# Moving two matmul groups of an expert's second layer behind a vote of the routing search

## The reference

```python
def _moe_ref(x, w_gate, w1, w2):
    ...
    logits = x @ w_gate
    order = np.argsort(-logits.flatten())
    for idx in order:
        tok, e = (int(idx) // E, int(idx) % E)
        if assigned[tok] >= 0 or counts[e] >= cap:
            continue
        assigned[tok] = e
        counts[e] += 1
    ...
    for e in range(E):
        mask = assigned == e
        h = np.maximum(x[mask] @ w1[e], 0.0)
        out[mask] = h @ w2[e]
```

## Time and profile before

| | |
|---|---|
| median of 3 runs | 1320.37 us (1319.72 to 1323.32) |
| profiled execution: its time, its span | 1320.37 us, 1318.5 us |
| PE matmul busy | 1231.4 us (93% of the span) |
| DVE busy | 914.4 us (69%) |
| ACT busy | 572.1 us (43%) |
| POOL busy | 286.2 us (22%) |
| L789 `combine` on PE | 576 matmuls, 156.5 us, 409 ns each |
| L715 `count` on PE | 1176 matmuls, 37.5 us |

### The profile page before, as it was taken

The page is one execution under the profiler, slowest core; times in us unless marked ns, Lnnn a source line. Parts: engine busy times, 40 slices in busy tenths (PEclk is TensorE's granted clock), DMA queues, the critical chain, the costliest instruction groups (busy, mean ns, idle before and its releaser), DMA issues.

```text
span 1318.5 us, 27799 instructions
## 1 busy us (share of the span) xinstructions
PE 1231.4 (93%) x9680; PEld 1096.5 (83%) x9680; DVE 914.4 (69%) x1818; ACT 572.1 (43%) x1224; POOL 286.2 (22%) x346
## 2 busy tenths in 40 slices
PE   7999983299999999999999999999999999999997
PEld 6888872278787787888898999989999898999986
DVE  4777765887887888765696666666666666766662
ACT  4666650123333233344415544544455444544541
POOL 4000000202202102120213323324233242333322
PEclk9999995589999999999999999999999999999999
DMA  7878744433332432543315233233333423334210
GB/s 146 169 169 163 166 97 182 153 113 109 125 120 70 147 133 65 194 147 107 110 34 192 72 107 111 81 104 106 126 123 120 144 79 104 100 125 135 88 43 13
DMA packets 174298, 154.65 MB, mean 117 GB/s; under 512 B 105117, under 2 KB 137885, under 8 KB 174240
## 3 DMA queue, kind: packets, MB, share of 16 engines
q1 hardware_dynamic: 151552, 102.83, 27.8%
q0 software_dynamic: 16128, 44.56, 11.0%
q10 hardware_dynamic: 6560, 6.49, 1.4%
HBM read 206.13 MB, written 33.75 MB: 182 GB/s over the span
## 4 chain that ended last, share of the span: by engine, by line
PE 38%; issue 37%; DVE 10%; POOL 9%; DMA 3%; ACT 1%; POOLq 1%; DVEq 0%; SPq 0%; ACTq 0%
PE bank L789 8%; PE bank L769 8%; DMA out<-result,token_now 3%; PE bank L645 3%; POOL partial L421 3%; POOL out L431 3%; PE bank L654 2%; PE bank L633 2%; POOL held L401 2%; PE bank L1001 2%; PE bank L669 2%; POOL x L405 2%; PE bank L715 2%; PE bank L1028 2%; PE bank L754 1%
## 5 line engine op out<-in xcount | busy, mean ns | idle before, releaser
L572 DVE TENSOR_TENSOR w_part<-w_sb,w_part 128x1024 fp32r<-128x1024 f32 x280 | 341.7, 1224 | 97.1 <-ACT w_part L566 89.1
L566 ACT CAST w_part<-w_sb 128x1024 fp32r<-128x1024 f32 x280 | 290.6, 1046 | 205.1 <-PE bank L1028 152.2
L1001 PEld LDWEIGHTS bank<-x2T,w_part 128*128 128x128 f32 x2688 | 326.3, 192 | 4.6 <-DVE x2T L1558 1.6
L1001 PE MATMUL bank<-x2T,w_part 128*128 128x256 f32 x2688 | 327.9, 283 | 1.8 <-DVE x2T L1558 1.8
L1028 PE MATMUL bank<-w_part,h2T 128*128 128x512 f32 x1344 | 312.6, 391 | 0.0
L1028 PEld LDWEIGHTS bank<-w_part,h2T 128*128 128x128 f32 x1344 | 250.2, 188 | 51.0
L789 PE MATMUL bank<-w_part,hT 128*128 128x512 f32 x576 | 156.5, 409 | 3.7 <-DVE w_part L572 3.7
L769 PE MATMUL bank<-xgT,w_part 128*128 128x384 f32 x768 | 146.5, 344 | 0.9 <-DVE xgT L1222 0.9
L1913 ACT ACTIVATE h2T<-bank 128x512 fp32r<-128x512 f32 x112 | 66.9, 598 | 180.4 <-PE bank L1001 141.3
L379 POOL DMA_INDIRECT xg<-x_dram,token_of x24 | 29.6, 1232 | 507.0 <-DVE token_of L1258 266.0
L769 PEld LDWEIGHTS bank<-xgT,w_part 128*128 128x128 f32 x768 | 133.6, 191 | 2.9 <-DVE xgT L1222 1.4
(11 more groups left out here) (281 smaller groups left out, 1306.2 us busy)
## 6 DMA issues: line engine op xcount, KB each, us to landing
w_sb<-in_moe_w SPq DMA_DIRECT2D x280, 512.0 KB
k_in<-in_k SPq DMA_DIRECT2D x32, 240.0 KB
v_in<-in_v SPq DMA_DIRECT2D x32, 240.0 KB
q_in<-in_q SPq DMA_DIRECT2D x32, 192.0 KB
x_dram<-x_sb SPq DMA_DIRECT2D x32, 192.0 KB, 3.1
out<-zeros SPq DMA_DIRECT2D x1, 6144.0 KB, 19.7
y_dram<-y_sb ACTq DMA_DIRECT2D x24, 256.0 KB, 2.0
x<-y_dram,slot_now POOLq DMA_INDIRECT x56
```

The costliest lines, as they stand in the source:

```text
L566: scalar.copy(split_part(0, c), raw_part(c)).then_inc(hi_ready[c], 1)
L572: nc.vector.tensor_tensor(split_part(1, c), raw_part(c), split_part(0, c).bitcast(F32), ALU.subtract).then_inc(lo_ready[c], 1)
L1001: last = nc.tensor.matmul(bank[2 + g % 2][:, at:at + TILE], w1_part[a][:, kt, f * P:(f + 1) * P], x2T[b][:, kt, :], start=(f % 2 == 0 and ...
```

## The change

Two numbers of each of two tuples of equal length differ. Of the 24 groups, groups 18 and 19 move from before the vote of round 5 to behind it, and group 20 moves from before the count of round 6 to behind it. Nothing is added or removed.

```diff
             def step(n, k, j):

-                before_votes = (0, 6, 9, 12, 15, 20, 22)
-                after_votes = (3, 8, 11, 14, 17, 21, 24)
+                before_votes = (0, 6, 9, 12, 15, 18, 22)
+                after_votes = (3, 8, 11, 14, 17, 20, 24)
                 done = 0
                 for s in range(len(SHIFTS)):
                     count(n, s)
```

## The result

The kernel after takes 1328.9 us (median of 7 runs, 1327.67 to 1332.73) against 1320.37 us for the kernel before (7 runs, 1319.41 to 1323.32): a ratio of 1.0063, 95% interval 1.0049 to 1.0079, so slower by 0.5 to 0.8%. The forecast was 1326.4 with a range of 1321.6 to 1327.8: the direction was right, the loss was larger, and the time is 1.1 us outside the range. The profiled execution of after took 1327.07 us with a span of 1325.2.

A forecast was written before the change was run, and what follows sets the result against it. PE was taken to bound each pass, with `met` of round 5 held. Six matmuls moved (1.39 us) less 0.18 us gained gives 1.21 us per pass, 6.05 in five, on 1320.37: 1326.4 us, range 1321.6 to 1327.8.

The forecast's parts named there:

- PE's row is unbroken and `met` is held: Rounds 5 and 6: PE has no idle time, while `met` of round 5 starts about 1.9 us after its count.
- the lead of vote 5: Round 5: the vote starts earlier than before the change, by a mean of 0.18 us over the five passes.
- The clock is cost at nothing too: PE in the passes: granted clock stays at 1.00 despite the new idle spots, so no time is added.
- the sum: Five passes: the vote of round 6 comes 1.21 us later in each, 6.05 us in total, giving 1326.4 us.
- The hold as tied to POOL's indirect DMAs: Round 5: POOL's series of indirect DMAs delays the count's update about 1.9 us; its end stays at the same moment.
- rival 1: Round 5: the count's update comes in time and PE's row stays unbroken, 1320.4 us; chance 0.10.
- Rival 3: Without a hold, the vote comes 1.39 us earlier and DVE carries that lead to the pass's end, 1313.4 us; chance 0.02.
- The edit behind the count: Round 6: group 20 behind the count adds 0.70 us of PE work, with `met` still hidden.

The follow-up runs named there:

- the delayed kernel: The changed kernel with two more operations on DVE right before `met` of round 5, writing what nobody reads; 1330.76 us, ratio 1.0092 against the kernel before.

## Why the prediction was right, and where it failed

**PE's row is unbroken and `met` is held: right for the profiled execution, and the mechanism of the loss was right.** PE idle before the vote of round 5 was put at 1.24 us and measured as 1.11 to 1.16; the lead of vote 5 was put at 0.18 (the five passes of before give 0.19) and measured as 0.18 to 0.21; vote 5 to vote 6 came out at 5.97 to 6.06 us for 5.97 where the clock stayed.

**"The clock is cost at nothing too: it stays at 1.00 in passes that already hold PE idle spots of 0.8 us": this step failed.** The term was worth 1.6 us a stretch, 3.1 to 3.2 us in the profile of the first comparison, and not 0. The mechanism of the sum was right; a term was sized at zero. The argument went from spots of 0.8 us, which the rows had, to one of 1.1 to 1.2 us behind the small matmuls of a count, which they had not. An edit that opens a spot longer than any in the passes needed a bound from a row at the other level, and there was one: in before's stretch at 638.3 the granted clock is 0.51, and nine matmuls take 3.70 us for 2.36 in the earlier trace rows, so a stretch costs between 1.3 and 1.7 us (half of 3.41). That stretch had no idle spot ahead of it, so the trace spoke against taking the clock for granted even in an unbroken row. Two such stretches give 1326.4 + 3.2 = 1329.6, and a range that held them would have held 1328.9.

**The hold as tied to POOL's indirect DMAs: right as to the source, and half of the truth.** It goes when three of the six are moved (1.0076 against 1.0006, on one chip). But the same six in the same place hold nothing on other chips. The forecast took it for a property of the program, "the same place in the same program", and gave its absence 0.10 as rival 1. That rival's number, 1320.4, is what the chips without the hold give: 1319.77 and 1318.74, level with their before. By the runs here both cases are common: two comparisons with after unaltered had the hold and two had not. A trace of one execution can't tell that; its evidence for the hold was good, and good for that execution only. That the comparison with the result had the hold too was luck for the forecast: on the two others its 1326.4 would have been some 7 us too long.

The Trainium skill (TensorE: Matmul & The Clock Gate, The cost: per-tile semaphore tail) was weighed in the prediction against the row of round 5. Its formula has a third term, 4.7 ns for each tile, that the prediction left out; for one matmul it changes nothing at this scale. The runs show both: with `met` at 411.87 behind a count that ends at 411.84 the trace agrees with its tail of some tens of ns, and with 1.99 us of "remote" it does not. The same page of the Trainium skill (HAM oscillation — how this bites in real kernels) describes a kernel whose matmul engine waits about 3 to 5 us for its next input again and again and falls back to the half clock each time. The idle spots here are much shorter, 1.0 to 1.3 us, and half clock followed all the same in 2 of 5 and 4 of 5 passes; read beforehand, the section would not have warned against the term of zero.

**Rival 3, faster through an early vote, was rightly put aside.** Where there is no hold, vote 5 does come 1.39 us earlier against vote 4 (4.09 us for 5.48), and vote 6 comes as much later against vote 5 (5.97 for 4.58). DVE's lead is lost before the tail of the pass, as argued from the earlier trace rows.

**The edit behind the count, by itself,** was put in the prediction at its own 0.70 us with no wait of its own. Alone it brings one: it costs 0.35 us a pass when groups 18 and 19 stay, by the wait for `xgT`, and nothing in the whole change, whose six matmuls behind the first transposes leave PE no such wait.

Three things stay open. Why the update is held in some comparisons and not in others was not tried. One chip (6) had no hold in any of its three comparisons and one (1) had none in its only one; another (14) had it in its only one, and the chip of the first comparison isn't on record. So that it belongs to the chip, and not to the time or the session, is likely and not shown. The medians stand 8.5 and 9.4 us over the medians of before, and the profiled executions 6.7 and 7.4 over these; the number of half-clock stretches in a run without a profile can't be seen, and one or two more of them, at 1.6 us each, would account for the difference. And what decides between full and half clock is open: in the delayed kernel the idle spot of 1.31 us in pass 4 was followed by full clock and the one of 1.20 us in pass 2 was not, and before's stretch at 638.3 came without any.

```profile
418.98 0.17 PE L722 MATMUL bank<-met,digit_unit 32*128 32x8 bf16 x1 [1.31 <-DVE met L1387]
```

## What to carry to other kernels

Work that stands in front of a wait can be a cover that the fast execution doesn't show: the same nine matmuls are needless on one chip and hide a late update on another, so take them away only with room for the latest arrival that any profile has shown. When a change opens an idle spot on PE, price it twice, once as the time itself and once with the work behind it at the lower clock, for which a stretch already at that level in the trace gives the size. And a kernel that gains or loses through one late semaphore should be timed on more than one chip before the number is believed.

## What the hardware showed

- An update of PE's semaphore is taken up by DVE 1.7 to 1.9 us behind the end of its matmul, beside a series of six indirect DMAs of POOL, in the first comparison and on one chip, and at once (0.03 us) on two others, with the same program and the same order.
- With three of the six moved away, it is taken up at once on that chip too, while five waits of ACT there still show "remote" (14.5 us of idle time in all).
- An idle spot of 1.0 to 1.3 us on PE was followed by a stretch of 3.41 us at half clock in 2, 2 and 4 of five passes; it costs 1.3 to 1.6 us where PE sets the pace (7.32 to 7.67 us from vote 5 to vote 6, for 6.03 to 6.04). With the spot filled there was none, nor in any of the other profiles without the spot.
- The kernel before has a half-clock stretch of its own at about 638 us, with PE busy for all of the 4.3 us before it. In another profile of the same kernel the same place runs at full clock, nine matmuls in 2.30 us for 3.70.
